# Weight loads in halves beside the last chunks of a scan, and a new order at three stage borders, on one Trainium2 core

## The reference

```
# attention: q, k, v, a_re, a_im of shape (4, 8, 768, 48)
scale = minimum(mag, 0.999) / (mag + 1e-6);  a = (a_re, a_im) * scale
for t in range(768):
    S_re, S_im = a_re*S_re - a_im*S_im + k_t v_t^T,  a_re*S_im + a_im*S_re
    y_t = q_t @ S_re                      # per batch and head
x = y as (3072, 384)
# soft mixture: phi (384, 32), 8 experts with 4 slots, w1 (8, 384, 1024), w2 (8, 1024, 384)
logits = x @ phi;  d = softmax(logits over tokens);  c = softmax(logits over slots)
slot_out[e] = relu((d.T @ x)[e] @ w1[e]) @ w2[e];  x = c @ slot_out
# network: w_in (384, 2048), w_out (2048, 384)
out = relu(x @ w_in)**2 @ w_out
```

## Time and profile before

| | us |
|---|---|
| median of 3 runs | 668.25 |
| lowest, highest | 667.24, 670.85 |
| the profiled execution | 667.75 |
| its span, first to last instruction | 666.0 |
| TensorE busy | 517.3 (78%) |
| VectorE busy | 418.1 (63%) |
| ScalarE busy | 324.4 (49%) |
| GpSimd busy | 147.8 (22%) |

### The profile page before, as it was taken

The page is one execution under the profiler, slowest core; times in us unless marked ns, Lnnn a source line. Parts: engine busy times, 40 slices in busy tenths (PEclk is TensorE's granted clock), DMA queues, the critical chain, the costliest instruction groups (busy, mean ns, idle before and its releaser), DMA issues.

```text
span 666.0 us, 11747 instructions
## 1 busy us (share of the span) xinstructions
PE 517.3 (78%) x4538; PEld 396.1 (59%) x4538; DVE 418.1 (63%) x680; ACT 324.4 (49%) x563; POOL 147.8 (22%) x128
## 2 busy tenths in 40 slices
PE   2000039796597977997887999989999999999996
PEld 1000016675375755775666874548888888888885
DVE  4799998979969999997734315167533333232331
ACT  5774135383455736332222332267665555565652
POOL 6001000100001000010000000036655555555653
PEclk9655569798797987998987999999999999999999
DMA  6400084724926434688698699900010101010101
GB/s 252 142 1 0 3 221 99 151 76 104 245 48 136 115 86 91 132 273 208 189 256 233 132 424 423 434 11 1 1 48 0 49 0 48 1 48 1 44 5 47
DMA packets 39558, 79.59 MB, mean 119 GB/s; under 512 B 7120, under 2 KB 28752, under 8 KB 37200
## 3 DMA queue, kind: packets, MB, share of 16 engines
q1 hardware_dynamic: 36192, 62.33, 33.1%
q10 hardware_dynamic: 3312, 16.52, 7.5%
HBM read 55.12 MB, written 4.72 MB: 90 GB/s over the span
## 4 chain that ended last, share of the span: by engine, by line
PE 53%; DVE 22%; DMA 9%; issue 6%; ACT 4%; SPq 4%; POOL 0%; ACTq 0%; DVEq 0%; POOLq 0%
PE ps L1248 10%; PE ps L1250 10%; PE ps L1249 10%; DMA stk<-xout 8%; PE ps L992 8%; SPq L253 4%; PE ps L1230 3%; DVE big L670 3%; DVE xout L791 2%; DVE tt L695 2%; DVE big L700 2%; PE ps L978 2%; PE ps L1150 2%; PE ps L1172 2%; DVE big L659 2%
## 5 line engine op out<-in xcount | busy, mean ns | idle before, releaser
L962 DVE TENSOR_TENSOR qs<-rs 128x512 f32<-128x512 f32 x96 | 75.1, 782 | 129.2 <-ACT rs L563 129.2
L626 POOL TENSOR_TENSOR hlo<-qs,hhi 128x512 fp32r<-128x512 f32 x96 | 126.9, 1322 | 125.4 <-DVE qs L962 122.0
L992 PE MATMUL ps<-stk 112*128 112x224 f32 (+1 forms) x384 | 94.3, 412 | 53.4 <-DMA stk<-xout 53.3
L978 PE MATMUL ps<-ident 128*32 128x512 bf16 x246 | 71.2, 391 | 69.0 <-DVE xout L791 69.0
L992 PEld LDWEIGHTS ps<-stk 112*128 112x128 f32 x384 | 83.2, 237 | 66.4 <-DMA stk<-xout 59.7
L1248 PE MATMUL ps<-hhi,who 128*128 128x512 f32 x288 | 112.1, 389 | 1.6 <-POOL hlo L626 1.6
L1250 PE MATMUL ps<-hhi,wlo 128*128 128x512 f32 x288 | 112.0, 389 | 0.0
L1249 PE MATMUL ps<-hlo,who 128*128 128x512 f32 x288 | 112.0, 389 | 0.0
L563 ACT ACTIVATE rs<-ps 128x512 f32<-128x512 f32 x96 | 57.5, 599 | 83.7 <-PE ps L1230 83.6
L978 PEld LDWEIGHTS ps<-ident 128*32 128x32 bf16 x246 | 19.3, 96 | 88.9 <-DVE xout L791 69.3
L613 POOL MEMSET big<- 128x2304 f32 x4 | 8.2, 2038 | 266.1 <-DVE big L700 266.1
(11 more groups left out here) (155 smaller groups left out, 811.3 us busy)
## 6 DMA issues: line engine op xcount, KB each, us to landing
stk<-xout SPq DMA_DIRECT2D x144, 128.0 KB, 3.6
wt<-in_w SPq DMA_DIRECT2D x10, 1536.0 KB, 12.3
xq<-in_xq SPq DMA_DIRECT2D x24, 384.0 KB, 4.3
wt<-in_w ACTq DMA_DIRECT2D x6, 1536.0 KB, 10.4
big<-in_a_all ACTq DMA_DIRECT2D x9, 768.0 KB, 4.8
vr<-in_v_all SPq DMA_DIRECT2D x24, 192.0 KB, 4.0
out<-ost SPq DMA_DIRECT2D x6, 768.0 KB, 3.5
wins<-in_w_in SPq DMA_DIRECT2D x1, 3072.0 KB, 17.4
```

Of the source, the lines that this page charges most:

```text
L626: pool.tensor_tensor(hlo[:, i % NHS, :], qs[:, i % NQS, :], hhi[:, i % NHS, :].bitcast(F32), ALU.subtract).then_inc(lo_ready, 1)
L962: dve.tensor_tensor(qs[:, i % NQS, :], rs[:, i % NQS, :], rs[:, i % NQS, :], ALU.mult).then_inc(sq_ready, 1)
L978: nc.tensor.matmul(ps[P - SL:P, bank, :], idb[:, 0:SL], idle, start=True, stop=True)
L992: last = nc.tensor.matmul(ps[:, h // 2, h % 2 * SK:h % 2 * SK + cols], x[:, 0:CH], x[:, CH:CH + cols], start=True, stop=True)
```

## The change

It has four parts.

1. The last three early weights (k = 6, 1, 3) are loaded in halves of 768 KB, one half beside each of chunks 18 to 23, in place of three whole loads beside chunks 18, 19 and 20. Their readers wait for 32 in place of 16.
2. In the last chunk's iteration (n = 23) pair 10 is done, `outputs(23)` follows behind it, ahead of `turn_x(22)` and `logits(22)`; pair 11 moves from iteration 26 to 25, and one iteration goes. Waits of `turn_x` and `flip` follow that order.
3. The first u block is copied and corrected alone, the other three between the first blocks of the last stage; `split_w` moves from ahead of the ReLU of a block to behind the square of the one before. `gate(1)` waits for one block in place of three, and the blocks' banks are 1, 5, 6, 7. `project` runs its six matmuls with the high part first and waits for the low part only then.
4. The last block of the last tile goes bank by bank; each bank is copied and stored (256 KB) as soon as it is done.

```diff
-        U_BANK = [5, 6, 1, 7]
+        U_BANK = [1, 5, 6, 7]
...
+        def pair_at(n):
+
+            if n >= NT - 1:
+                return {NT - 1: NT // 2 - 2, NT + 1: NT // 2 - 1}.get(n)
+            return n // 2 - 2 if n >= 4 and n % 2 == 0 else None
...
+        LOADED = [32 if k in EARLY[3:] else 16 for k in range(2 * NX)]
...
-            for t in range(TT):
+            for t in range(TT - 1):
                 sp.wait_ge(acc_copied, KM * (t + 1))
...
+            t = TT - 1
+            for k in range(KM):
+
+                if k == 1:
+                    sp.wait_ge(end_dve, 1)
+                else:
+                    sp.wait_ge(end_act, 1 + k // 2)
+                sp.dma_start(out[k * P:(k + 1) * P, t * TW:(t + 1) * TW], ost[:, t % 2, k]).then_inc(stored_last, 16)
...
+            def load_half(i):
+
+                k, half = EARLY[i // 2], slice(i % 2 * KM * FE // 2, (i % 2 + 1) * KM * FE // 2)
+                src = (w2 if k % 2 else w1)[k // 2].rearrange("p a b -> p (a b)")
+                act.dma_start(wt[k][:, half], src[:, half]).then_inc(ld_w[k], 16)
...
-                    if p == B and c < 3:
+                    if p == B and c < NC:
...
-                        load_w(EARLY[3 + c])
+                        load_half(NC + c)
...
-                    if 1 <= n <= NT:
+                    if 1 <= n < NT:
                         copy_y(n - 1)
...
+                    if n == NT - 1:
+                        copy_y(n)
...
-            for b in range(4):
+
+            def copy_u(b):
                 act.wait_ge(u_done, b + 2)
...
+            copy_u(0)
+            split_w(0)
             for i in range(TT * F2B + 1):
-                if i < F2B:
-                    split_w(i)
...
+                if i < 3:
+                    copy_u(i + 1)
+                if i < F2B - 1:
+                    split_w(i + 1)
...
+            for k in (0, 2):
+                act.wait_ge(end_done, k + 1)
+                nc.scalar.activation(ost[:, t % 2, k, :], ps[:, 2 + 3 * (t % 2) + k, :], ACT.Copy).then_inc(end_act, 1)
...
-                    if n >= 4 and n % 2 == 0:
-                        running_max(n // 2 - 2)
+                    if n < NT - 1 and pair_at(n) is not None:
+                        running_max(pair_at(n))
                     if 1 <= n <= NT:
                         apply_mask(n - 1, 0)
                         apply_mask(n - 1, 1)
+                    if n == NT - 1:
+                        running_max(pair_at(n))
...
+            low_u(0)
...
+                if i < 3:
+                    low_u(i + 1)
...
-                    pe.wait_ge(et_copied, (m - 1) // 2 * 2)
+                    pe.wait_ge(et_copied, NT - 2 if m == NT - 2 else (m - 1) // 2 * 2)
...
-            for n in range(NT + 3):
+            for n in range(NT + 2):
...
-                if 1 <= n <= NT:
+                if 1 <= n < NT:
                     keep_busy(1)
                     outputs(n - 1)
...
                     weighted_sums(pair)
+                if n == NT - 1:
+                    outputs(n)
...
                 if i == 1:
-                    pe.wait_ge(u_low, 3)
+                    pe.wait_ge(u_low, 1)
...
+                if i == TT * F2B - 1:
+
+                    pe.wait_ge(lo_ready, i + 1)
+                    for k in range(KM):
+                        nc.tensor.matmul(accs[k], wh[k], hi, start=False, stop=False)
+                        nc.tensor.matmul(accs[k], wh[k], lo, start=False, stop=False)
+                        nc.tensor.matmul(accs[k], wl[k], hi, start=False, stop=True).then_inc(end_done, 1)
+                    return
+                for k in range(KM):
+                    nc.tensor.matmul(accs[k], wh[k], hi, start=(f == 0), stop=False)
+                    nc.tensor.matmul(accs[k], wl[k], hi, start=False, stop=False)
                 pe.wait_ge(lo_ready, i + 1)
                 for k in range(KM):
-                    nc.tensor.matmul(acc, wh, hi, start=(f == 0), stop=False)
-                    nc.tensor.matmul(acc, wh, lo, start=False, stop=False)
-                    last = nc.tensor.matmul(acc, wl, hi, start=False, stop=(f == F2B - 1))
+                    last = nc.tensor.matmul(accs[k], wh[k], lo, start=False, stop=(f == F2B - 1))
```

More of the change, by code:

```diff
@@ L226, in program @@
         stored = [sem(f"stored{k}") for k in range(2)]
+        end_done, end_act, end_dve, stored_last = sem("end_done"), sem("end_act"), sem("end_dve"), sem("stored_last")
         block = ctx.enter_context(nc.Block())
@@ L310, in _ @@
                   .then_inc(stored[t % 2], 16)
-            for k in range(2):
-                sp.wait_ge(stored[k], 16 * TT // 2)
+            t = TT - 1
[5 more added lines that the diff above has]
+                sp.dma_start(out[k * P:(k + 1) * P, t * TW:(t + 1) * TW], ost[:, t % 2, k]).then_inc(stored_last, 16)
+            sp.wait_ge(stored[0], 16 * TT // 2)
+            sp.wait_ge(stored[1], 16 * (TT // 2 - 1))
+            sp.wait_ge(stored_last, 16 * KM)
         @block.scalar
@@ L470, in _ @@
             for p in range(B + 1):
-                for c in range(NC + 3 * (p == B)):
+                for c in range(NC + 2 * (p == B)):
                     n = (p - 1) * NC + c
@@ L497, in _ @@
                                 inv_mag(p + 1, t)
-                    pair = n // 2 - 2 if n >= 4 and n % 2 == 0 else None
+                    pair = pair_at(n)
                     if pair is not None:
@@ L571, in _ @@
                     copy_out(t - 1, 1)
-            copy_out(TT - 1, 0)
-            copy_out(TT - 1, 1)
+            t = TT - 1
+            act.wait_ge(stored[t % 2], 16 * (t // 2))
+            for k in (0, 2):
+                act.wait_ge(end_done, k + 1)
+                nc.scalar.activation(ost[:, t % 2, k, :], ps[:, 2 + 3 * (t % 2) + k, :], ACT.Copy).then_inc(end_act, 1)
         @block.gpsimd
@@ L942, in _, with low_u @@
             dve.tensor_copy(so[:], ps[:, 4, 0:KM * SL].rearrange("p (k s) -> p k s", k=KM)).then_inc(so_ready, 1)
-            for b in range(4):
+            def low_u(b):
                 dve.wait_ge(u_high, b + 1)
@@ L965, in _ @@
                     copy_out(t - 1)
-            copy_out(TT - 1)
+            t = TT - 1
+            dve.wait_ge(stored[t % 2], 16 * (t // 2))
+            dve.wait_ge(end_done, 2)
+            dve.tensor_copy(ost[:, t % 2, 1, :], ps[:, 2 + 3 * (t % 2) + 1, :]).then_inc(end_dve, 1)
         @block.tensor
@@ L1066, in flip @@
                 pe.wait_ge(exp_done, m // 2 + 1)
-                pe.wait_ge(x_copied, min(m // 2 * 2 + 3, NT))
+                pe.wait_ge(x_copied, m // 2 * 2 + (2 if m >= NT - 4 else 3))
                 if m == NT - 1:
@@ L1142, in hidden @@
                 for e in (2 * p, 2 * p + 1):
-                    pe.wait_ge(ld_w[2 * e], 16)
+                    pe.wait_ge(ld_w[2 * e], LOADED[2 * e])
                 if p >= 2:
@@ L1164, in slot_outputs @@
                 for e in (2 * p, 2 * p + 1):
-                    pe.wait_ge(ld_w[2 * e + 1], 16)
+                    pe.wait_ge(ld_w[2 * e + 1], LOADED[2 * e + 1])
                 pe.wait_ge(h_ready, p + 1)
@@ L1242, in project @@
                 pe.wait_ge(hi_ready, i + 1)
+                hi, lo = hhi[:, i % NHS, :], hlo[:, i % NHS, :]
+                accs = [ps[:, 2 + 3 * (t % 2) + k, :] for k in range(KM)]
+                wh = [who[:, f, k * P:(k + 1) * P] for k in range(KM)]
+                wl = [wlo[:, f, k * P:(k + 1) * P] for k in range(KM)]
+                if i == TT * F2B - 1:
[8 more added lines that the diff above has]
+                    nc.tensor.matmul(accs[k], wl[k], hi, start=False, stop=False)
                 pe.wait_ge(lo_ready, i + 1)
                 for k in range(KM):
-                    acc = ps[:, 2 + 3 * (t % 2) + k, :]
-                    wh, wl = who[:, f, k * P:(k + 1) * P], wlo[:, f, k * P:(k + 1) * P]
-                    hi, lo = hhi[:, i % NHS, :], hlo[:, i % NHS, :]
-                    nc.tensor.matmul(acc, wh, hi, start=(f == 0), stop=False)
-                    nc.tensor.matmul(acc, wh, lo, start=False, stop=False)
-                    last = nc.tensor.matmul(acc, wl, hi, start=False, stop=(f == F2B - 1))
+                    last = nc.tensor.matmul(accs[k], wh[k], lo, start=False, stop=(f == F2B - 1))
                 last.then_inc(acc_done, 1)
```

## The result

| | before, us | after, us |
|---|---|---|
| median of 12 executions | 668.14 | 663.79 |
| lowest, highest | 664.14, 670.85 | 661.03, 668.35 |
| the profiled execution | 667.75 | 665.93 |
| its span | 666.0 | 664.2 |

The changed kernel takes 0.9941 of the time before, with a 95% interval of 0.9915 to 0.9967. It is 4.35 us faster by the medians, where 5.75 were forecast, counted from the profiled 667.75. Of the kernels tried further down, one execution of part 1 alone (674.99 us, over 1.5% above the fastest of that kernel) is left out of its ratio.

What follows compares the result with a forecast made beforehand. Bound taken: TensorE, held up by late stacks and slow clock at chunks 19 and 20, then DMA saturated up to k = 14. 667.75 - 8.6 + 3.65 + 2.0 - 1.5 - 1.3 = 662.0 us; range 655 to 667.5.

Steps and rivals of the forecast that it cites:

- rival C: Chunk 20: the pile-up stays in part, chunk 21 starts only 4.6 us earlier; 666.0 us, chance 0.18.
- rival E: Each half load keeps a fixed 1.8 us no queue hides, 3.6 us more ahead of k = 14; 665.6 us, chance 0.05.
- The chunks: Chunks 19 and 20: halves cut waits and slow clock, so chunk 21 starts 8.6 us earlier; bounds 10.1 and 4.6.
- chunk 20's stack: Scores of chunk 20: with halves, TensorE waits 0 to 3 us for this stack, taken as 1.1.
- Rival D: Chunks: a load delays a stack by the same 5.6 us whatever its size, so slower; 670.6 us, chance 0.12.
- slack of 4.4 us for the stack of chunk 23: This stack lands 4.4 us before its need, covering the 2 to 3 us a half delays it.
- Bytes ahead of k = 14: Behind the chunks: two halves of k = 3 put 3.65 us of bytes ahead of k = 14; bounds 2 to 4.5.
- Slow clock at hidden(3): After the wait in front of hidden(3) the clock falls, costing 2.0 us; bounds 0 and 2.5.
- Part 2: Last chunk's new order gains 0.8 us, bounds 0 and 1.2, but counts nothing as hidden(3) waits for DMA.
- First blocks: Start of the last stage: project(0) 2.5 us earlier, 1.0 given back; gain 1.5 us, bounds 0.8 and 2.3.
- Tail: Last tile: 0.5 us less copying and 0.8 from a smaller final store; gain 1.3 us, bounds 0.4 and 1.7.
- what would have shown it wrong: Either hidden(3) shows no wait, or chunk 20 still waits over 3 us.

Runs made afterwards that it cites:

- part 1 alone: The kernel before with only the six half loads beside chunks 18 to 23 and their waits; 668.09 us, 0.9968 of before.
- shifted halves: The changed kernel with the half load beside chunk 19 moved to chunk 21, which then has two; 663.00 us, one execution.
- filler: The changed kernel with 24 matmuls that compute nothing put ahead of hidden(3); 659.00 us, one execution.
- hidden(3) later: The changed kernel with TensorE doing slot_outputs(1) and transpose_h(2) ahead of hidden(3), loads unaltered; 660.17 us.
- parts 2 to 4: The changed kernel with the three whole loads back beside chunks 18, 19 and 20; 665.21 us, 0.9951 of before.
- k = 13 behind 14: The changed kernel with the load of k = 13 issued behind that of k = 14 instead of ahead; 660.23 us, 0.9871 of before.
- both orders: The changed kernel with k = 13 loaded behind k = 14 and hidden(3) moved behind slot_outputs(1) and transpose_h(2); 659.24 us.
- both orders and shifted halves: The kernel of both orders with the half load beside chunk 19 moved to chunk 21; 661.35 us.

## Why the prediction was right, and where its terms were off

The sign, the place and the chain of causes held: the chunks get faster, k = 14 then sets hidden(3), and the last stage and the tail gain. The median of after, 663.79, lies 1.8 us above the 662.0 that was forecast, within the range. But the sizes held less well than the total. Part 1 as a whole was forecast to gain 8.6 - 3.65 - 2.0 = 2.95 us; the pair of profiles has a loss of 1.8, and part 1 alone comes to 0.9968 of before, 2.1 us less, with an interval that holds no change. Parts 3 and 4 gave 3.6 where 2.8 were forecast. That the total still came near is in part luck, and the time alone doesn't tell the forecast (662.0) from rival C (666.0) or E (665.6): the profiled execution took 665.93. The terms one by one:

**The chunks, forecast 8.6 us.** In the profile of after it is 6.0 from chunk 18 to 21 (36.84 - 30.79), and 5.1 on the clock of the whole run, because chunk 18 itself began 0.95 later (332.63, and in before the row below), ahead of the first half, which goes out at 332.82.

```profile
331.68 3.29 PE L992 MATMUL ps<-stk 112*128 112x224 f32 x16 [1.88 <-DMA stk<-xout]
```

The term that was off is chunk 20's stack: a wait of 1.1 us was taken and 2.27 came, and the slow clock behind it, 1.69 us, stood in the lower bound alone. The range given for the wait, 0 to 3, covers it; "nearer the lower end" was the wrong choice, because the half beside chunk 19 holds this stack up, as the shifted halves show. Where the wait was short (filler 0.81, part 1 alone 0.98, hidden(3) later 1.52) the clock held and the forecast was met: 9.35, 8.9 and 8.65 us less. In the profile of after it is rival C's case (4.6 us) more than the forecast.

**Rival D** (a delay that doesn't depend on the size) falls. From issue to landing the stacks of chunks 19 and 20 took 8.0 to 10.4 us at the median beside whole loads (before, and parts 2 to 4); the stack of chunk 20 took 6.4 beside a half, in after:

```profile
stk<-xout SPq DMA_DIRECT2D x6, 128.0 KB, 6.4
```

Its other loss came in small. The prediction counted on a slack of 4.4 us for the stack of chunk 23. With the half of chunk 22 beside it the last of its six transfers lands 9.2 us after its issue in after (4.7 before), at about 382.6 us, and the scores start at 382.82; the slack is used up. In part 1 alone chunk 23 waits 0.31 us for it. Chunk 23 starts 10.67 us behind chunk 22 in after, 0.9 more than before (9.74), and this has a second cause that nobody forecast: TensorE stands still from 381.74 to 382.38 in the middle of the logits matmuls, where the program has no wait. The trace's packets have one of 16 KB on the instruction queue that ends at 380.98, 1.40 us before TensorE goes on. The same stall stands in k = 13 behind 14, filler and both orders, each time 1.37 to 1.41 us behind the end of such a packet. It looks as if TensorE waits there for its next instructions; no run tested that.

**Bytes ahead of k = 14, forecast 3.65 us, bounds 2 to 4.5.** Measured 5.5 in after and 3.9 to 4.9 in halves shifted, part 1 alone, hidden(3) later and filler (landings of 41.9 to 42.9 us behind T); so the upper bound was too low for most. The windows at 372 to 380 us show one reason: DMA is busy at a share of 0.92 to 1.12 but moves 221 to 234 GB/s, half of the 427 at 412 to 416, while the stack of chunk 23 goes through beside the weights. Before has such a stretch too, but a shorter one. In windows of 2 us behind T it moved 198, 281 and 430 GB/s, and after 243, 224 and 235. The difference is 0.4 MB, about 1.0 us at the full rate. So the mixing accounts for about 1.0 of the 1.9 us that came on top of the bytes in after, and the other 0.9 stays open. Leaving k = 3 out takes away both the bytes and the longer mixing, so a fixed cost of each half (rival E, 1.8 us each) is not separated from it; what came on top of the bytes, 0.3 to 1.9 us for two halves, is below the 3.6 of that rival. The Trainium skill, page DMA: Bandwidth & Descriptors, section Rules for kernel authors, asks for transfers of 1 MiB or more. No run here shows what the smaller size costs: one whole weight of 1536 KB taken from ahead of k = 14 brought 43.4 - 38.7 = 4.7 us, 1.1 above its bytes, and so no less than the halves.

**Slow clock at hidden(3), forecast 2.0 us.** 1.42 in after, 2.37 with the halves shifted and 2.57 with part 1 alone; within the bounds of 0 to 2.5 but for 0.07 in the last.

**Part 2, forecast nothing.** Right for after: hidden(3) waits for DMA whatever comes before it. Its size, 0.8 forecast, is 0.95 where chunk 23 follows at the old distance (hidden(3) later reaches hidden(0) 24.95 us behind T, before 25.90). In after the late start of chunk 23 has already used it up (25.89).

**First blocks, forecast 1.5 us.** Measured 1.9: the last stage takes 226.09 in place of 228.01 us, and 226.05 to 226.08 in eight other kernels. project(0) starts 2.7 us earlier against 2.5 forecast, and of the 1.0 that was to be given back, 0.8 was. The low part is indeed late, by this line of the waits (us in total, times, longest):

```profile
PEld ps L1306 <- POOL hlo L660: 1.4, 4, 0.5
```

**Tail, forecast 1.3 us.** Measured 1.7: the stores land 2.1 us behind their issue at the median and not 3.4, so the whole 1.3 us of the smaller store came, where 0.8 was taken.

Of what would have shown it wrong, neither came: hidden(3) waits, and chunk 20 waits under 3 us. The wait at hidden(3) was forecast at 4.4 us, and 5.56 came.

The sum by the measured terms is +1.8 - 1.9 - 1.7 = -1.8 for the pair of profiles, and -4.35 for the medians. The difference is not settled row by row. It most likely lies in the chunks, where the start of chunk 18 alone varies from 330.53 to 337.89 us over the profiles shown, and chunk 20's wait from 0.81 to 2.34 us in kernels with a half beside chunk 19.

## What to carry to other kernels

When a stall ahead of a full transfer queue is removed, ask for each transfer behind it whether it is in the critical order: here 5 to 9 us of saved waiting were turned into a wait of 5.56 us at the first weight that had no slack, and moving one load behind it gave more than the whole first part, by the medians. Bytes put ahead of a late transfer cost more than the full rate says when they mix with small transfers: here 3.9 to 5.6 us for 3.65 us of bytes. And when a load is cut up to spare a transfer beside it, look at what each piece stands beside: here the one half beside chunk 19 made the 0.8 to 2.3 us of waiting at chunk 20.

## What the runs showed of the hardware that was not expected

The length of a wait alone doesn't tell whether the clock falls behind it. Scores ran in 4.98 us after a wait of 1.73 us (k = 13 behind 14, chunk 20) and in 3.29 after one of 2.12 (both orders and shifted halves, chunk 22); hidden(3) kept 2.78 after 1.56. Even the same wait in the same code goes both ways: behind the 1.59 us ahead of project(0) the matmuls kept the full clock in before and took 0.63 us in place of 0.39 in the profile of part 1 alone, which made its last stage 1.6 us longer. In the 5 us from the product with w_in on, TensorE had been busy for 4.89 us in the one and 4.88 in the other. No run varied what TensorE did before a wait, so what decides stays open.

hidden(0) can start at the low level without a long wait ahead of it: in part 1 alone TensorE was busy for 3.42 of 4 us at 396 to 400, and the granted clock was 0.78 there and 0.86 in the next 6 us (windows):

```profile
396.00:400.00 4.00, 3.42 (x24) 2.02 (x25) 1.33 (x4) 0.49 (x1) 0.29 (x1) 0.78 1.00 421
400.00:406.00 6.00, 6.00 (x50) 2.88 (x43) 3.68 (x6) 1.44 (x2) 0.00 (x0) 0.86 1.01 426
```

It came in four of the ten experiments (part 1 alone, parts 2 to 4, both orders, both shifted). The busy time doesn't tell these from the others: after was busy for the same 3.42 us in the same stretch, 396 to 400, with a granted clock of 1.00, and before for 3.42 us in the last 4 us ahead of its hidden(0), also with 1.00.

The mean granted clock of an execution doesn't rank its time: of after, the shortest execution (661.03 us) had 0.901 and the longest (668.35) 0.946.
